# Attention, SoLU and hard-swish layers on one core: the first batch written out engine by engine, weight pieces cast by GpSimd and their remainders moved

## The reference

```python
# 1. attention in chunks of 32 queries; keys: 8 memory keys + the window c-16 .. c+32+8
scores = scale * np.matmul(q_c, k_full.transpose(0, 1, 3, 2))
a = np.exp(scores - np.max(scores, axis=-1, keepdims=True))
out[:, :, c_start:c_end] = np.matmul(a / (np.sum(a, axis=-1, keepdims=True) + 1e-09), v_full)
# 2. x is 3072 x 512, w_in 512 x 1024, w_out 1024 x 512
h = x @ w_in
e = np.exp(h - np.max(h, axis=-1, keepdims=True))
solu = h * (e / (np.sum(e, axis=-1, keepdims=True) + 1e-09))
x = ((solu - mean) / np.sqrt(var + 1e-06) * g_ln) @ w_out
# 3. w_in 512 x 2048, w_out 2048 x 512
h = x @ w_in
out = (h * np.clip(h + 3.0, 0.0, 6.0) / 6.0) @ w_out
```

## Time and profile before

| what | value |
|---|---|
| time, median of 3 runs | 938.34 us (937.13 to 939.4) |
| profiled execution: its own time | 938.23 us |
| its span, first to last instruction | 936.4 us |
| mean granted clock of PE over the span | 0.985 |
| PE busy | 905.9 us (97%) |
| DVE busy | 685.4 us (73%) |
| ACT busy | 473.2 us (51%) |
| POOL busy | 273.0 us (29%) |
| first instruction of batch 1 on PE | 82.41 us after the span's start |

### The profile page before, as it was taken

One profiled execution on the slowest core, in us unless ns is written; L12 is line 12 of the kernel. 1 busy time (PEld: TensorE's weight loads), 2 busy tenths in 40 slices (PEclk: granted clock), 3 DMA queues, 4 the chain that ended last, 5 costly groups with the idle time before them and its releaser, 6 DMA issues.

```text
span 936.4 us, 17274 instructions
## 1 busy us (share of the span) xinstructions
PE 905.9 (97%) x6200; PEld 812.0 (87%) x6200; DVE 685.4 (73%) x1094; ACT 473.2 (51%) x1092; POOL 273.0 (29%) x324
## 2 busy tenths in 40 slices
PE   7887999999999999999999999999999999999998
PEld 7666888988888888889988888888799999999997
DVE  3898687878777777866686555555788988878783
ACT  4645465555656564635675555455654333333320
POOL 5452165554432343552002332323550000000000
PEclk8987999999999999999999999999999999999999
DMA  9633326666644476458463333332987434344441
GB/s 191 149 67 63 93 53 178 180 179 171 190 141 137 100 219 165 139 175 334 170 254 128 116 138 123 142 127 111 351 315 270 137 101 149 114 141 135 130 137 45
DMA packets 146907, 146.46 MB, mean 156 GB/s; under 512 B 96936, under 2 KB 107176, under 8 KB 145832
## 3 DMA queue, kind: packets, MB, share of 16 engines
q1 hardware_dynamic: 134328, 100.55, 37.0%
q0 software_dynamic: 7920, 38.94, 11.5%
q10 hardware_dynamic: 4608, 6.29, 1.9%
HBM read 90.05 MB, written 55.71 MB: 156 GB/s over the span
## 4 chain that ended last, share of the span: by engine, by line
PE 80%; DVE 13%; DMA 3%; ACT 2%; issue 2%; SPq 0%; POOL 0%; DVEq 0%; POOLq 0%
PE banks L873 25%; PE banks L916 21%; PE banks L1057 21%; PE banks L827 3%; PE banks L840 2%; PE banks L864 2%; PE banks L796 2%; DVE prob L1317 2%; PE banks L853 2%; DVE gs_raw L1474 2%; DVE gs L1293 2%; DVE small L1313 1%; DMA k_in<-in_k_dram 1%; DMA ws<-w_split_scratch 1%; DVE score L1301 1%
## 5 line engine op out<-in xcount | busy, mean ns | idle before, releaser
L1057 PE MATMUL banks<-vs,gs 128*128 128x256 f32 x2016 | 243.3, 283 | 2.7 <-DVE o_stage L1507 1.5
L1057 PEld LDWEIGHTS banks<-vs,gs 128*128 128x128 f32 x2016 | 242.3, 192 | 3.8 <-DVE o_stage L1507 1.7
L916 PE MATMUL banks<-xs,ws 128*128 128x512 f32 x1008 | 230.5, 390 | 2.4 <-DMA ws<-w_split_scratch 1.8
L916 PEld LDWEIGHTS banks<-xs,ws 128*128 128x128 f32 x1008 | 188.3, 188 | 43.2 <-DMA ws<-w_split_scratch 2.2
L1253 ACT CAST gs<-gs_raw 128x1792 fp32r<-128x1792 f32 x48 | 81.6, 1700 | 132.2 <-DVE gs_raw L1474 132.1
L873 PE MATMUL banks<-y_t,w_out 128*128 128x384 f32 x768 | 140.8, 337 | 0.0
L873 PE MATMUL banks<-w_in,x_t 128*128 128x512 f32 x552 | 133.2, 397 | 1.1 <-DVE solu L1347 1.1
L873 PEld LDWEIGHTS banks<-y_t,w_out 128*128 128x128 f32 x768 | 132.2, 188 | 0.7
L873 PEld LDWEIGHTS banks<-w_in,x_t 128*128 128x128 f32 x552 | 103.1, 190 | 23.1 <-DVE solu L1347 1.4
L1105 ACT ACTIVATE prob<-score,small 96x128 f32<-96x128 f32 x256 | 99.8, 397 | 18.2 <-DVE small L1306 18.2
L1474 DVE TENSOR_TENSOR gs_raw<-gs_raw 128x256 f32<-128x256 f32 x192 | 82.6, 431 | 29.4 <-DMA gs_raw<-g_scratch 24.3
(11 more groups left out here) (88 smaller groups left out, 1077.4 us busy)
## 6 DMA issues: line engine op xcount, KB each, us to landing
g_scratch<-part SPq DMA_DIRECT2D x96, 256.0 KB, 2.0
gs_raw<-g_scratch SPq DMA_DIRECT2D x45, 512.0 KB, 3.9
q_in<-in_q_dram SPq DMA_DIRECT2D x32, 192.0 KB, 3.9
x_scratch<-x_out ACTq DMA_DIRECT2D x32, 192.0 KB, 2.0
out_dram<-o_stage SPq DMA_DIRECT2D x12, 512.0 KB, 5.7
k_in<-in_k_dram SPq DMA_DIRECT2D x24, 240.0 KB
v_in<-in_v_dram SPq DMA_DIRECT2D x24, 240.0 KB
v_split_scratch<-v_split POOLq DMA_DIRECT2D x3, 1792.0 KB, 7.7
```

Source lines behind the costliest of these rows:

```text
L916: mm = pe.matmul(ps, ws[:, W_OF[i], a, kc, :], xs[g][X_OF[i]][:, m, kc, :], start=(fresh and x == 0), stop=(x == len(passes) - 1), skip_gr ...
L1057: mm = pe.matmul(m_ps[i][:, s, :], gs[x][:, a, G_OF[i], s * P:(s + 1) * P], vs[p][:, m, V_OF[i], :], start=(p == 0 and s == 0 and y == 0), ...
```

## The change

Only the first batch and the weights are touched; the loop's instructions stay the same, but for SP, where q of a tile is loaded as soon as its slot's q has been turned (before: once its k had been turned too). Each engine gets a function `first_batch` that lists the steps of the first batch in an order of its own, in half tiles. The diff, cut to its core:

```diff
-        w_raw = at("w_raw", 184, [P, 2, PIECE], F32)
+        w_first = at("w_first", 184, [P, 2, PIECE], F32)
+        w_later = at("w_later", 112, [P, 6, PIECE], F32)
...
             def load_weights(p):
-                s = p % 2
+                if p < 2:
+                    pool.wait_ge(k_in_here[0], kv_here(0, 0))
+                else:
+                    pool.wait_ge(w_raw_here[p % 2], 16 * (p // 2))
...
+                nc.gpsimd.tensor_copy(w_split_at(p, HI), w_piece(p)).then_inc(w_hi_done, 1)
+
+            def low_weights(p, x):
+                if x == 0:
+                    pool.wait_ge(w_hi_done, p + 1)
+                    pool.wait_ge(w_lo_done, p)
+                cs = slice(x * PIECE // 4, (x + 1) * PIECE // 4)
+                piece = nc.gpsimd.tensor_tensor(w_split_at(p, LO)[:, cs], w_piece(p)[:, cs],
+                                                w_split_at(p, HI)[:, cs].bitcast(F32), ALU.subtract)
+                if x == 3:
+                    piece.then_inc(w_lo_done, 1)
...
+            def first_batch():
+                pool.wait_ge(k_in_here[0], kv_here(0, 0))
+                with nc.allow_non_contiguous_dma(reason="one vector, once"):
+                    pool.dma_start(g_ln, moe_g_ln.rearrange("(c p) -> p c", p=P)).then_inc(g_ln_here, 16)
+                load_weights(0)
+                load_weights(1)
...
+            def hidden_part(m, x):
+                half, ks = x // 2, 2 * (x % 2)
...
+                if m == 0 and half == 0:
+                    pe.wait_ge(w_lo_done, ks + 2)
...
+            def first_batch():
+                pe.wait_ge(ident_ready, 1)
+                keep_busy(8)
+                turn_q(0, early_ps[0])
...
+            def first_batch():
+                load_window(act, k_in, k, mem_k, k_in_here, 0, 0)
+                act.wait_ge(three_ready, 1)
+                nc.scalar.copy(hsum, three)
+                copy_q(0, early_ps)
...
+            def low_weights(p):
+                dve.wait_ge(w_hi_done, p + 1)
+                low(w_split_at(p, LO), w_piece(p), w_split_at(p, HI)).then_inc(w_lo_done, 1)
```

More of the change, by code:

```diff
@@ L373, in _ @@
         def _(sp):
[L374 to L393, removed]
-                for t in range(TILES):
[L395 to L401, removed]
+            def load_v(b, t):
+                n = TILES * b + t
+                if type(n) is not int or n >= 2:
+                    sp.wait_ge(av_done, n - 1)
+                load_window(sp, v_in, v, mem_v, v_in_here, b, t)
@@ L403, in batch @@
+            def batch(b):
+                for t in range(TILES):
+                    load_q(b, t)
+                    load_k(b, t)
                     if t > 0:
[L404 to L408, removed]
+                        load_v(b, t - 1)
+                    else:
+                        load_v(b - 1, TILES - 1)
+            first_batch()
@@ L552, in split_weights, with high_weights @@
+            def high_weights(p):
                 if p < WP1:
-                    hi, lo = (w_in[:, a, p, :] for a in (HI, LO))
+                    pool.wait_ge(w_raw_here[p % 2], 16 * (p // 2 + 1))
                 else:
[L555 to L560, removed]
@@ L838, in turn_probs @@
                         pe.wait_ge(y_lo_done, 2 * MPG * (NG - 1))
[L839 to L842, removed]
+                    turn_half(n, half)
             def attend(b, t, very_first):
@@ L897, in hidden @@
+                for half in range(2):
+                    mm = split_products(h_ps[:, half * BANK:(half + 1) * BANK],
+                                        lambda a, kc: x_t[:, par, a, kc, u * P:(u + 1) * P],
+                                        lambda a, kc: w_in[:, a, kc, half * BANK:(half + 1) * BANK], KD)
                 mm.then_inc(h_done, 1)
@@ L947, in batch @@
+            def batch(b, last=False):
                 for kk in range(TILES):
-                    w = work(kk, first, last)
+                    w = work(kk, last)
                     n = TILES * b + kk - 1
                     i, ii, u = 2 * b + kk // TPG, kk // TPG, kk % TPG
-                    early = first and 1 <= kk <= TPG
-                    if first and kk == 0:
-                        turn_early_qk(0)
-                    if w["own"] and not early:
-                        turn_qk(b if kk else b - 1, (kk - 1) % TILES, first, i, u)
+                    if w["own"]:
+                        turn_qk(b if kk else b - 1, (kk - 1) % TILES, i, u)
@@ L964, in batch @@
                         begin_next(4, 3, acc_ps[0], False)
[L965 to L969 removed]
                     if w["before"]:
                         turn_probs(n - 1, w["own"])
[L972 removed]
+                    if w["own"]:
                         scores(n, False)
                     if w["turn"]:
[L975 removed]
+                        turn_ln(turned_tile(i, u), u, 2 * n if w["before"] else 2 * NA)
                     if last and kk == TPG:
@@ L1173, in batch @@
+            def batch(b, last=False):
                 for kk in range(TILES):
-                    w = work(kk, first, last)
+                    w = work(kk, last)
                     n = TILES * b + kk - 1
                     i, ii, u = 2 * b + kk // TPG, kk // TPG, kk % TPG
-                    if first and kk < TPG:
-                        copy_qk(kk, early_ps)
-                    if first and kk == 0:
-                        act.wait_ge(w_raw_here[0], 16)
-                        nc.scalar.copy(w_in[:, HI, 0, :], w_raw[:, 0, :]).then_inc(w_hi_done, 1)
@@ L1196, in batch @@
                         high_x(n - 1, (kk - 2) % TPG, (kk - 2) // TPG % 2)
-                    if kk >= TPG if first else not last:
-                        copy_qk(n + 1, turn_ps)
+                    if not last:
+                        copy_qk(n + 1)
                     if w["mm1"]:
@@ L1393, in batch @@
                     if w["own"]:
-                        max_scores(n, {0: 2, 1: 0}.get(kk, 1), first and kk == 1)
-                    if first and kk == 0:
-                        dve.wait_ge(w_hi_done, 1)
-                        low(w_in[:, LO, 0, :], w_raw[:, 0, :], w_in[:, HI, 0, :]).then_inc(w_lo_done, 1)
+                        max_scores(n, {0: 2, 1: 0}.get(kk, 1))
                     if w["turn"]:
@@ L1429, in _ @@
             dve.wait_ge(mask_ready, 1)
-            batch(0, first=True)
+            first_batch()
             with dve.Fori(1, B) as b:
```

612 lines of the change are left out of this document (493 added, 119 removed).

## The result

The changed kernel takes **949.23 us** (median of 4 runs, 947.26 to 950.25) against 938.85 (4 runs beside them): ratio 1.0111, 95% interval 1.009 to 1.0133. It is slower by about 10 us, where 928 was forecast. The profiled execution spans 947.3 us.

What follows compares the result with a forecast made beforehand. DVE was taken to pace the first batch and PE the rest. Start -2.0, lows +3.4, order -3.9, stalls -5.7 and idle -1.9 sum to -10.1 us, from 938.23 to 928 us; range 921.5 to 934.5, likeliest 925 to 930.5.

Steps and rivals of the forecast that it cites:

- that PE goes on from there as before: After DVE's last row of the first batch, PE was assumed to continue unchanged, so the gain there stays: -10.1 us.
- what starts earlier there ends earlier: From 98.4 to 900 us PE is the bound, busy 793.27 of 801.60 us, so an earlier start gives an earlier end.
- if the loop's own pace has changed: Sign of being wrong: the loop behind the first batch no longer takes the same time as before within 1 us.
- Start, -2.0: DVE's first row, a mask, comes at 8.9 us instead of 10.94 because k tile 0 lands earlier; bounds 0 and -3.
- later than 10: Sign of being wrong: DVE's first mask, forecast near 8.9 us, comes after 10 us.
- Lows, +3.4: DVE takes over the low parts of w_in pieces 1 to 3, 1.14 us each, in the first batch: +3.4 us.
- Stalls, -5.7: DVE rows held up by POOL's rows in the first batch: 13.8 us of stall falls to 8.1; bounds 10 and 4.
- Order, -3.9: Fewer DVE rows in the first batch directly follow the row they use, 18 instead of 57: -3.9 us, bounds 0 and -5.
- Idle, -1.9: DVE's first-batch waits for ACT shrink from 8.3 to 2.0 us, and a new wait for w_in piece 0 adds 4.4.
- until about 15: Sign to look for: DVE idle until about 15 us before its first low part, that of w_in piece 0.
- more: Rival: larger gain, 920 to 924 us, from a shorter piece 0 wait, fewer stalls and batch 1 at full clock; chance 0.18.
- The clock: Rival: with fewer `ident` matmuls PE's clock drops around the first batch, giving back 3 to 7 us: 930.5 to 935; chance 0.20.

Runs made afterwards that it cites:

- both loops held: Changed kernel with 36 one-column matmuls on PE ahead of the loop, plus 24 instructions on ACT (924.6 us) or k tile 0's loads back on SP (924.12 us).
- five starts tried: Instructions by which ACT's loop starts later than in the kernel before: 0 (that kernel), 2 (924.12 us), 5 (changed kernel, 949.23), 13 (938.29), 29 (924.6).
- before with 5 on ACT: Kernel before with 10 waits on an already raised semaphore, packed into 5 instructions, on ACT ahead of the first batch: 957.28 us (ratio 1.0201).
- changed with PE's filler: Changed kernel with 36 one-column matmuls that do nothing, on PE alone ahead of the loop: 940.78 us (ratio 1.0027).

## Why the prediction was wrong

**The step that failed** is the assumption "that PE goes on from there as before", and under it "what starts earlier there ends earlier". PE did bound that stretch, and none of its matmuls changed; but the loop's pace did, at its two jumps back, by 22.6 us. The prediction named it as a sign of being wrong ("if the loop's own pace has changed") and gave no mechanism a chance. None of the rivals was it: what made the kernel slower was no edit's wait, but how many instructions stand ahead of the loop. With both loops held the changed first batch gave 924.6 and 924.1 us, within the stated range of 921.5 to 934.5 and below the 928: what the prediction had wrong by itself in the first batch is small beside what it left out.

How the loop is held is worked out, not shown. In straight code (700 to 930 us after) 15 packets of queue 8 came for 1869 matmuls, 125 each with as many weight loads; so a packet is about 256 instructions, and PE's body (768 matmuls, as many loads, about 105 others by its program) about 6.4 packets. If the second stall, some 60 instructions into the body, marks a packet's end, the body lies on 8 packets in the changed kernel. In the kernel before it starts 143 instructions later and has 7 waits fewer (PE's loop did not stay the same to the instruction: the two waits ahead of each turn of the probabilities changed places, and 7 more waits became instructions of their own), and lies on 7. The Trainium skill (Advanced Engine Details and Errata, "ISA Cache") gives TensorE 128 KB and a line of 16 KB; that makes 8 lines, an estimate, since the same list says "Only 2 cache lines!". By 8 lines, 7 packets and one fetched ahead fit, 8 and one don't; the runs agree with that, and not with 2. The Trainium skill also says that a jump out of the present two pages must fetch its target (Runtime: NRT & Kernel Launch, "Instruction fetch mechanics"). Of PE that is not so here: before, it jumps back six blocks and fetches nothing. ACT's packets are 8 KB by the profile's page (0.16 MB in 19), thus 128 instructions of the size that PE's have, and its 281 instructions lie on 3 or 4. The five starts tried (held at 0, 2 and 29, not at 5 and 13) fit a body that is held on 3 and not on 4, if the kernel before starts it 99 to 101 instructions into a packet; no run shows where it does.

**The other steps**, from DVE's groups in the first batch of the changed kernel, 10.74 to 71.26 us, as in the earlier trace rows:

```profile
L1586 DVE TENSOR_TENSOR prob<-prob,small 96x512 f32<-96x512 f32 x14 | 11.6, 832 | 0.2
...
L1576 DVE TENSOR_SCALAR small<-small 96x4 f32<-96x4 f32 x14 | 3.3, 233 | 1.0 <-ACT prob L1298 1.0
...
L1547 DVE TENSOR_TENSOR w_in<-w_first,w_in 128x1024 fp32r<-128x1024 f32 x2 | 2.4, 1208 | 2.9 <-POOL w_in L608 2.9
```

- *Start, -2.0*: -0.2. The k tile did come early (turned at 6.77, not 8.60), but a q turn stands between it and the scores, which ran at half the clock (2.02 us, 1.73 before) and ended at 10.58; the first mask came at 10.74, not 8.9. By the prediction's own sign ("later than 10") this step was wrong.
- *Lows, +3.4*: four at about 1.21 us against one, +3.6.
- *Stalls, -5.7*: the two groups take 14.9 us instead of 25.9, -11.0; 20 was forecast. The stall left is 11.6 - 14 x 0.69 + 3.3 - 14 x 0.17 = 2.9 us, below the lower bound of 4. The mean over arrivals counts a wait for each row; in the trace 6 of the 28 rows were held up by over 0.2 us. Whether the quarters or the rows between did that wasn't tried.
- *Order, -3.9*: the durations of DVE's rows sum to 60.8 us in 53.90 busy, 68.6 in 65.57 before; overlap grew by 3.9.
- *Idle, -1.9*: 60.52 - 53.90 = 6.6 us, 10.7 before: -4.1. The wait for piece 0 ended at 15.54 as forecast ("until about 15"), but was 2.9 us, since DVE came later (4.4 was entered for it, where the prediction's own working gives 4.3).

Together -15.6 us; DVE's last row comes 15.95 earlier and PE's `hidden` 15.3. The direction of each term held, and the sum was that of the rival "more". Of the 3.7 us that the prediction priced for DVE's lows holding up POOL's casts, 0.6 came: DVE's low at 22.31 overlaps a cast that took 1.61 us instead of 1.04. The Trainium skill has the two engines share a port pair that one instruction locks for its whole length (SBUF — State Buffer, "SBUF: two separate sides"); this pair of rows agrees.

```profile
22.31 1.19 DVE L1547 TENSOR_TENSOR w_in<-w_first,w_in 128x1024 fp32r<-128x1024 f32 x1
```

```profile
22.79 1.61 POOL L608 CAST w_in<-w_later 128x1024 fp32r<-128x1024 f32 x1 [3.76 <-DMA w_later<-in_moe_w_in_dram]
```

*The clock*: 0.92 in DVE's first batch, 0.86 before, with 14 `ident` matmuls instead of 52; that rival fell.

## What to carry to other kernels

A loop's cost can hang on the number of instructions ahead of it. Before a change that adds or removes some, look at the packets of the instruction queues during the loop: where there are none, the loop is held, and whether it stays so is to be tested with filler ahead of it. An engine that stands on "issue" ahead of the first row behind a jump, or within a row of like instructions without a wait, may be waiting for its program. "issue" alone doesn't say so: PE's 7.81 us ahead of the turns of ln had that mark and were a wait for ACT.

## What was not expected of the hardware

- One stall of PE for its program is 2.8 to 3.5 us, with two at the first jump. ACT's is longer: 7.69, 8.45 and 8.57 us between its rows at the first jump and 5.27, 5.16 and 5.04 at the second (changed kernel, before with 5 on ACT, changed with PE's filler), where 0.97 and 0.94 stand in the kernel before. Whether the transfers of that time make it longer wasn't tried.
- The price was 14.6 to 19.7 us for two jumps on one engine, more than the stalls themselves; behind them other engines wait and TensorE's granted clock falls to half (0.74 on the mean from 172 to 198 us). Of the 19.7 a part lies behind the loop (5.9 in the profiled execution).
- PE and ACT lose their loops independently, each with its own queue (8 and 14) and its own border.
